# An mLSTM kernel takes its first log rows by products in place of row transfers, and its later logs behind the second unit

## What is computed

```
for t in range(S):
    m_new = maximum(f[t] + m, i[t])
    f_stab, i_stab = exp(f[t] + m - m_new), exp(i[t] - m_new)
    m = m_new
    C = f_stab * C + i_stab * outer(v[t], k[t])
    n = f_stab * n + i_stab * k[t]
    y[t] = sigmoid(o[t]) * (C @ q[t]) / max(|n @ q[t]|, 1)
x = y as (1536, 320)
x = sum over 4 experts e of p[:, e] * (relu(x @ w1[e]) @ w2[e])     # F = 1024
out = ((x @ w_a) * (x @ w_b)) @ w_out                              # 1536 wide
```

## Time and profile before

| what | before |
|---|---|
| median of three runs | 607.03 us (605.69 to 608.39) |
| profiled execution, its own time | 606.54 us |
| its span in the profile | 604.5 us |
| TensorE busy (matmuls) | 597.0 us, 99% of the span |
| VectorE busy | 360.0 us, 60% |
| ScalarE busy | 293.7 us, 49% |
| GpSimd busy | 179.2 us, 30% |
| traffic | 38.38 MB, mean 63 GB/s |

### The profile page before, as it was taken

How to read it: one execution, slowest core, us unless ns; L and a number is a source line. 1 busy time by engine, 2 the same in 40 slices (tenths; PEclk the granted TensorE clock), 3 DMA queues, 4 the chain that set the end, 5 groups by cost and what they waited for, 6 DMA issues and landing times.

```text
span 604.5 us, 10937 instructions
## 1 busy us (share of the span) xinstructions
PE 597.0 (99%) x3991; PEld 581.0 (96%) x3991; DVE 360.0 (60%) x705; ACT 293.7 (49%) x622; POOL 179.2 (30%) x246
## 2 busy tenths in 40 slices
PE   7999999999999999999999999999999999999997
PEld 6888899999999999999999999999999999999997
DVE  7877984454474443644544635389796665666555
ACT  5888745424443344433344434656744543444332
POOL 3466430014340134200425101515035521553000
PEclk9999999999999999999999999999999999999999
DMA  4675541003311011410032100212102310120011
GB/s 128 200 227 183 166 127 51 11 1 69 97 40 62 1 47 23 137 40 23 0 71 87 57 12 1 47 25 87 57 12 47 108 58 12 42 51 1 1 67 65
DMA packets 21028, 38.38 MB, mean 63 GB/s; under 512 B 3520, under 2 KB 11280, under 8 KB 20976
## 3 DMA queue, kind: packets, MB, share of 16 engines
q1 hardware_dynamic: 19040, 35.02, 20.0%
q10 hardware_dynamic: 1936, 2.67, 1.3%
HBM read 26.42 MB, written 1.97 MB: 47 GB/s over the span
## 4 chain that ended last, share of the span: by engine, by line
PE 94%; DVE 4%; issue 1%; DMA 1%; ACT 0%; DVEq 0%
PE PS L1697 38%; PE PS L1616 12%; PE PS L1619 12%; PE PS L1617 12%; PE PS L1618 12%; PE PS L1559 3%; PE PS L1528 1%; PE PS L1516 1%; PE PS L1476 1%; PE PS L1502 1%; PE PS L1478 1%; PE PS L1542 1%; DMA dec_r<-llo 1%; DVE pt L1067 0%; DVE acc L1274 0%
## 5 line engine op out<-in xcount | busy, mean ns | idle before, releaser
L1697 PE MATMUL PS<-w2h,hh 128*128 128x320 f32 x528 | 164.9, 312 | 0.0
L1697 PE MATMUL PS<-w2l,hh 128*128 128x320 f32 x528 | 163.4, 310 | 0.0
L1697 PE MATMUL PS<-w2h,hl 128*128 128x320 f32 x528 | 163.2, 309 | 0.0
L1616 PE MATMUL PS<-xop,wop 128*128 128x384 f32 x400 | 138.5, 346 | 0.0
L1619 PE MATMUL PS<-xop,wop 96*128 96x384 f32 x400 | 135.0, 337 | 0.0
L1617 PE MATMUL PS<-xop,wop 128*128 128x384 f32 x400 | 134.8, 337 | 0.0
L1618 PE MATMUL PS<-xop,wop 128*128 128x384 f32 x400 | 134.6, 337 | 0.0
L734 ACT ACTIVATE hh<-c_s 128x384 fp32r<-128x384 f32 x120 | 62.8, 524 | 100.1 <-DVE c_s L1247 27.9
L1697 PEld LDWEIGHTS PS<-w2h,hh 128*128 128x128 f32 x528 | 99.5, 189 | 0.3 <-DVE hl L1224 0.2
L1697 PEld LDWEIGHTS PS<-w2l,hh 128*128 128x128 f32 x528 | 99.7, 189 | 0.0
L1697 PEld LDWEIGHTS PS<-w2h,hl 128*128 128x128 f32 x528 | 99.4, 188 | 0.0
(11 more groups left out here) (146 smaller groups left out, 803.5 us busy)
## 6 DMA issues: line engine op xcount, KB each, us to landing
s<-in_wt SPq DMA_DIRECT2D x24, 256.0 KB, 3.1
kvo<-in_tok SPq DMA_DIRECT2D x12, 480.0 KB, 4.2
wop<-t1h SPq DMA_DIRECT2D x48, 112.0 KB, 2.2
qk<-in_qk_t SPq DMA_DIRECT2D x24, 160.0 KB
s<-in_w SPq DMA_DIRECT2D x12, 320.0 KB, 2.9
wop<-t1l SPq DMA_DIRECT2D x24, 112.0 KB, 2.2
s<-in_w_out SPq DMA_DIRECT2D x12, 160.0 KB, 2.2
out_y<-acc SPq DMA_DIRECT2D x12, 160.0 KB, 1.9
```

The costliest lines, as they stand in the source:

```text
L1616: nc.tensor.matmul(to, ws[0], xs[0], start=opens, stop=False, skip_group_check=True)
L1697: got = nc.tensor.matmul(bank, left, (w2l if part == 1 else w2h)[p][:, f, :], start=opens and part == 0, stop=closes and part == 2)
```

## The change

Chunk 0's logs are computed first, on 128 columns, and then chunk 1's (`early_logs`). Units 0 and 1 get their row terms without transfers: `log_weights` adds, for each of the 8 heads of such a unit, one product of the head's selecting columns (`dec_r`, 64 partitions) with `lrow`, a tile whose partitions 0 to 15 hold the high and 32 to 47 the low rows. The four transfers of first rows go, and load_rows(2) waits for chunk 1's rows alone. The scan for the rest of the maxima moves behind weigh(0); rest_logs and rest_ends move behind take_num(0) and add_update(0) in unit 1, and normalise(0) behind weigh(2). The halves of m_r move: on SyncE behind load_rows(3), on ScalarE behind weights(1). On TensorE log_weights(0) comes ahead of products(0), log_weights(2) behind update(0), and turning the rest of the logs behind from_state(2); of 17 products of ones 10 stay. On GpSimd the step matrices of chunks 2 to 5 are made after chunk 1's rows, the mask before. load_kvo(1) comes right behind load_qk(1).

```diff
@@ -96,8 +96,9 @@
         li0 = sb("li0", [BH, EARLY], F32, inner)
-        lhi0 = sb("lhi0", [BH, EARLY], F32R, inner)
-        llo0 = sb("llo0", [BH, EARLY], F32R, inner)
+        lf0 = sb("lf0", [BH, P], F32, inner)
+        lrow = sb("lrow", [64, EARLY], F32R, inner)
+        lhi0, llo0 = lrow[0:BH, :], lrow[32:32 + BH, :]
         gate_r = sb("gate_r", [REST, 2, P], F32, inner)
@@ -121,7 +122,6 @@
         inter_s = [sb(f"inter_s{b}", [P, H, D1], F32, inner) for b in range(B)]
-        lf0 = wgt[B - 1][1][0:BH, 0:2, :].rearrange("r c t -> r (c t)")
         num = [sb(f"num{b}", [P, H, D1], F32, inner) for b in range(B)]
@@ -339,7 +339,7 @@
                 c, b = u // B, u % B
-                sp.wait_ge(rows_ready, 1 if c == 1 else 2)
+                sp.wait_ge(rows_ready, 2 if c == 1 else 3)
                 sp.wait_ge(dec_done, 2 * (u - B) + 2)
@@ -348,15 +348,9 @@
-            def load_first_high_row(b):
-
-                sp.wait_ge(rows_ready, 1)
-                sp.wait_ge(picked, 3 * b + 3)
-                sp.dma_start(f32(dec_r[b][64:65, :, :]), f32(lhi0[b * H:(b + 1) * H, 0:P])).then_inc(rows_in[b], 16)
-
             def load_dec_l(c):
-                sp.wait_ge(pool_const, 6)
+                sp.wait_ge(pool_const, 11)
                 sp.wait_ge(dec_l_ready, 1)
@@ -399,21 +393,19 @@
-            sp.dma_start(gate[:, :, 0:EARLY], gates[:, :, 0:EARLY]).then_inc(gates_in, 16)
-            sp.dma_start(gate[:, :, EARLY:S], gates[:, :, EARLY:S]).then_inc(rest_in, 16)
+            sp.dma_start(gate[:, :, 0:P], gates[:, :, 0:P]).then_inc(gates_in, 16)
+            sp.dma_start(gate[:, :, P:S], gates[:, :, P:S]).then_inc(rest_in, 16)
             sp.wait_ge(qk_zero, 1)
...
             load_qk(1)
-            load_first_high_row(0)
-            load_first_high_row(1)
-            sp.wait_ge(m_ready, 1)
-            sp.dma_start(m_r[:, 1, :], m[:, P + 1:S + 1]).then_inc(m_in, 16)
             load_kvo(1)
...
             load_rows(3)
+            sp.wait_ge(m_ready, 1)
+            sp.dma_start(m_r[:, 1, :], m[:, P + 1:S + 1]).then_inc(m_in, 16)
             load_qk(2)
@@ -456,12 +448,17 @@
             nc.gpsimd.memset(ones[:, :], 1.0).then_inc(pool_const, 1)
-            nc.gpsimd.memset(f32(dec_l[:, :, :]), 1.0).then_inc(pool_const, 1)
-            pool.wait_ge(pool_const, 5)
-
-            nc.gpsimd.affine_select(out=dec_l[:, :, :], in_=dec_l[:, :, :], compare_op=ALU.is_ge, fill=0.0, base=PICKED - 1,
-                                    pattern=[[0, NC], [1, P]], channel_multiplier=-1).then_inc(pool_const, 1)
-            pool.wait_ge(rows_ready, 1)
+            nc.gpsimd.memset(f32(lrow[:, :]), 0.0).then_inc(pool_const, 1)
+
+            def steps(cs):
+
+                nc.gpsimd.memset(f32(dec_l[:, cs, :]), 1.0).then_inc(pool_const, 1)
+                pool.wait_ge(pool_const, 6 if cs.start == 0 else 10)
+
+                nc.gpsimd.affine_select(out=dec_l[:, cs, :], in_=dec_l[:, cs, :], compare_op=ALU.is_ge, fill=0.0, base=PICKED - 1,
+                                        pattern=[[0, cs.stop - cs.start], [1, P]], channel_multiplier=-1).then_inc(pool_const, 1)
+
+            steps(slice(0, 2))
             nc.gpsimd.memset(mask[:, :, :], 0.0).then_inc(mask_ready, 1)
@@ -470,6 +467,9 @@
                 nc.gpsimd.memset(vx[b][:, :, D:D1], 1.0).then_inc(pool_const, 1)
+            pool.wait_ge(rows_ready, 2)
+            steps(slice(2, NC))
+            for b in range(B):
                 nc.gpsimd.memset(state[b][:, :, :, :], 0.0).then_inc(pool_const, 1)
@@ -656,12 +656,6 @@
-            def load_first_low_row(b):
-
-                act.wait_ge(rows_ready, 1)
-                act.wait_ge(picked, 3 * b + 3)
-                nc.scalar.dma_start(f32(dec_r[b][65:66, :, :]), f32(llo0[b * H:(b + 1) * H, 0:P])).then_inc(rows_in[b], 16)
-
             def take_v(u):
@@ -779,22 +773,20 @@
                 pick_heads(b)
-            for b in range(B):
-                load_first_low_row(b)
-            act.wait_ge(m_ready, 1)
-            nc.scalar.dma_start(m_r[:, 0, :], m[:, P:S]).then_inc(m_in, 16)
             weights(0)
...
             weights(1)
+            act.wait_ge(m_ready, 1)
+            nc.scalar.dma_start(m_r[:, 0, :], m[:, P:S]).then_inc(m_in, 16)
             gates_of(0)
...
                     weights(u + 1)
-                if u == 1:
+                if u == 2:
                     act.wait_ge(ex_turned, 2)
@@ -1082,7 +1074,7 @@
                 else:
-                    dve.wait_ge(pool_const, 10)
+                    dve.wait_ge(pool_const, 13)
                 for j in range(2):
@@ -1149,23 +1141,30 @@
-            def first_logs():
-                dve.wait_ge(dve_const, 1)
-                dve.wait_ge(pool_const, 4)
-                dve.wait_ge(gates_in, 16)
-                nc.vector.tensor_tensor_scan(m[:, 1:EARLY + 1], gate[:, 1, 0:EARLY], gate[:, 0, 0:EARLY], m[:, 0:1], ALU.add, ALU.max).then_inc(logs0, 1)
-                dve.wait_ge(logs0, 1)
-                n = logs_of(gate[:, 0, 0:EARLY], gate[:, 1, 0:EARLY], m[:, 0:EARLY], m[:, 1:EARLY + 1], lf0, lsum0[:, :], li0[:, :], lhi0[:, :],
-                            llo0[:, :], logs0, 1, True)
-                dve.wait_ge(pool_const, 6)
-                first_two = li0[:, :].rearrange("r (c t) -> r c t", c=2)
-                nc.vector.tensor_copy(dec_l[0:BH, 0:2, :], first_two).then_inc(logs0, 1)
+            def early_logs(c, n):
+
+                cols, ends = slice(c * P, (c + 1) * P), slice(c * P + 1, (c + 1) * P + 1)
+                if c == 0:
+                    dve.wait_ge(dve_const, 1)
+                    dve.wait_ge(pool_const, 5)
+                    dve.wait_ge(gates_in, 16)
+                else:
+                    dve.wait_ge(rest_in, 16)
+                nc.vector.tensor_tensor_scan(m[:, ends], gate[:, 1, cols], gate[:, 0, cols], m[:, c * P:c * P + 1], ALU.add, ALU.max).then_inc(logs0, 1)
                 dve.wait_ge(logs0, n + 1)
-                nc.vector.tensor_tensor(dec_l[32:32 + BH, 0:2, :], first_two, f32(dec_l[0:BH, 0:2, :]), ALU.subtract).then_inc(dec_l0_ready, 1)
+                n = logs_of(gate[:, 0, cols], gate[:, 1, cols], m[:, cols], m[:, ends], lf0[:, :], lsum0[:, cols], li0[:, cols], lhi0[:, cols],
+                            llo0[:, cols], logs0, n + 1, c == 0)
+                dve.wait_ge(pool_const, 7)
+                nc.vector.tensor_copy(dec_l[0:BH, c, :], li0[:, cols]).then_inc(logs0, 1)
+                dve.wait_ge(logs0, n + 1)
+                nc.vector.tensor_tensor(dec_l[32:32 + BH, c, :], li0[:, cols], f32(dec_l[0:BH, c, :]), ALU.subtract).then_inc(dec_l0_ready, 1)
+                return n + 1
+
+            def first_ends():
                 dve.wait_ge(dec_l0_ready, 1)
-
                 nc.vector.tensor_scalar(li0[:, 0:P], li0[:, 0:P], lsum0[:, P - 1:P], None, ALU.add).then_inc(ex_logs, 1)
-                dve.wait_ge(rest_in, 16)
+
+            def rest_maxima():
                 nc.vector.tensor_tensor_scan(m[:, EARLY + 1:S + 1], gate[:, 1, EARLY:S], gate[:, 0, EARLY:S], m[:, EARLY:EARLY + 1], ALU.add, ALU.max).then_inc(m_ready, 1)
@@ -1194,12 +1193,15 @@
-            first_logs()
+            logged = early_logs(0, 0)
+            first_ends()
+            early_logs(1, logged)
             for u in range(NU):
...
                 if u == 0:
-                    rest_logs()
-                    rest_ends()
+                    rest_maxima()
+                if u == B:
+                    normalise(0)
                 if u >= B:
@@ -1208,7 +1210,11 @@
                         x_low(0, u - 7)
-                    normalise(u - 1)
+                    if u == 1:
+                        rest_logs()
+                        rest_ends()
+                    else:
+                        normalise(u - 1)
                 if u == NU - 1:
@@ -1489,17 +1495,22 @@
                     pe.wait_ge(picked, 3 * b + 3)
-                    pe.wait_ge(pool_const, 6)
+                    pe.wait_ge(pool_const, 7)
+                    pe.wait_ge(rows_ready, 1)
+                else:
+                    pe.wait_ge(rows_in[b], 32 * c)
                 if c < 2:
-                    pe.wait_ge(dec_l0_ready, 1)
+                    pe.wait_ge(dec_l0_ready, c + 1)
                 else:
                     pe.wait_ge(dec_l_in[c], 32)
-                pe.wait_ge(rows_in[b], 32 * (c + 1))
                 pe.wait_ge(mask_ready, 3)
...
                     nc.tensor.matmul(PS[:, DEC + q, :], dec_l[:, c, :], dec_r[b][:, q:H:2, :], start=True, stop=False, skip_group_check=True)
+                    for p in range(NP if c == 0 else 0):
+                        nc.tensor.matmul(PS[:, DEC + q, p * P:(p + 1) * P], dec_r[b][0:64, 2 * p + q, :], lrow[:, 0:P], start=False, stop=False,
+                                         skip_group_check=True)
                 for q in range(2):
@@ -1534,7 +1545,7 @@
                 pe.wait_ge(vx_ready, u + 1)
-                pe.wait_ge(pool_const, 10)
```

(14 more changed lines are left out.)

## The result

The changed kernel took 621.71 us (median of six runs, 611.07 to 633.22) against 606.9 for the kernel before (six runs, 605.69 to 608.39). The ratio, which leaves out the runs above 1.5% over the fastest, is 1.0135 with a 95% interval of 1.0069 to 1.0202. The forecast was 608.3 us in a range of 605.0 to 610.8 and "no measurable change": wrong. The six times themselves are part of the result: 611.07, 615.01, 619.58, 623.83, 628.53, 633.22. The six runs of the kernel before have nothing like this spread.

A forecast was written before the change was run, and what follows sets the result against it. TensorE, busy for 99% of the span, was taken to bound the kernel; the start's gain was outweighed by products(3) coming 1.5 us late: 608.0 against the profiled run, 608.5 against the median, forecast 608.3 us, range 605.0 to 610.8.

The forecast's parts named there:

- Start: TensorE, unit 0: first limit ready at 6.45 us, log_weights(0) starts at 6.5 us, not 10.91.
- The added products: log_weights(0) and log_weights(1): 8 more products each at 0.11 us, making the part 1.8 us at high clock.
- What it uncovers: TensorE ahead of unit 3: log_weights(3) waits for unit 2's exponentials; a gain of 1.1 us is left of 4.4.
- The logs of the rest: VectorE: rest_logs starts at 16.2 us, not 13.69; dec_l_ready comes at 19.25, not 16.85, 2.4 us later.
- SyncE's queue: Behind dec_l_ready: 3.36 us of issue to load_qk(3) at 22.65, then 3.8 us; products(3) 1.5 us later.
- The mark: Start of products(3) on TensorE in unit 3: 26.45 us in place of 24.98, 1.5 us later.
- Afterwards TensorE's own work rules.: TensorE behind products(3): later loads add nothing more to the 1.5 us already lost.
- a rival with the clock in it: Clock low from 8.1 us to the end of log_weights(1): 2.5 us on top of +1.5, 610.8 us; chance 0.15.
- The dummy products: Units 0 and 1: seven products of ones gone, named only as a ground for the clock staying low.
- The port: VectorE's first logs: GpSimd's select and cast stop them for 0.9 us in all, 609.2 us; chance 0.1.
- The range: Whole kernel: 605.0 us, the gain's bottom, to 610.8 us, the clock's rival and run scatter.
- the first rival: SyncE does not bind, TensorE's own order decides: −1.1 us, 605.7 us, or −2.3 with cheaper added products; chance 0.25.

The follow-up runs named there:

- the two traces above: Changed kernel with 6 ones ahead of log_weights(4) and 7 ahead of products(3): 609.56 to 622.80 us; with the 6 alone: 609.60 to 621.43 us.
- the run with 622.80 us above: Profiled run of the changed kernel with 6 products of ones ahead of log_weights(4) and 7 ahead of products(3); its four runs: 609.56, 620.89, 622.74, 622.80 us.
- another kernel: Changed kernel with 13 products of ones at the start in place of 10, both waits of unit 3 left: 614.55 to 625.24 us in six runs.
- a third kernel: Changed kernel with only SyncE's order changed, load_kvo(2) and load_qk(3) ahead of load_dec_l(2): 608.03 us median of ten, ratio 1.0032.
- the last kernel: Changed kernel with rest logs early, SyncE's loads reordered, 13 ones at the start, and log_weights(2) ahead of outputs(0): 607.73 us against the kernel before, ratio 1.0035.

## Why the prediction was wrong, step by step

- **Start.** First log product at 7.04 for 6.5: VectorE's first logs ended at 6.77 for 6.45 (two of its operations were longer beside GpSimd's mask, the sums of 0.46 and 0.36 us that take 0.28 and 0.27 for chunk 1), and 0.27 us lie between. Right in kind.
- **The added products.** 0.147 us each for 0.11; they lie between the bounds of 0.068 and 0.213. With 8 to a unit that is 0.3 us a unit, and the wide product of each half took 0.43 from start to start in place of 0.34: 0.5 us a unit in all. In unit 0 that was hidden by luck. The forecast had the first 1.6 us at low clock, 0.8 us of loss, but in the profiled run the products were at full clock from the first on, so log_weights(0) took 2.33 us for 2.55. log_weights(1) had no such help: 2.36 us for 1.8. It ended at 12.98 for 12.1, outputs(0) at 15.98 for 15.0.
- **What it uncovers.** The wait for unit 2's exponentials came as said: 0.67 us at 18.06, for 0.45 expected at 16.8.
- **The logs of the rest.** `dec_l_ready` at 20.21 for 19.25, against 16.85 before. rest_logs took 2.96 us (3.05 expected) and started at 17.25 for 16.2, right behind add_update(0) (16.54 to 17.22), which waited for update(0): the 1 us by which the units were later. m_r was late as well, but did not bind in this run. The scan of the maxima took 1.70 us beside GpSimd in place of 1.27 (timeline of VectorE, below) and ended at 13.82 for 12.8; SyncE issued its half of m_r at 14.49, behind load_rows(3), and it landed 2.3 us after, at about 16.8.
- **SyncE's queue.** 3.38 us from `load_dec_l(2)` to `load_qk(3)` (20.28 to 23.66) for 3.36; products(3) 4.28 after that for 3.8. The mark came at 27.94 for 26.45, 3.0 us late in place of 1.5. Of the missing 1.5 us, 1.0 was `dec_l_ready` and 0.5 the transfer. The mechanism, its place and its order were right; the size was half.
- **"Afterwards TensorE's own work rules."** This is the step that failed. It carried the shift at full clock to the end, and I had priced the waits of unit 3 as waits only. They cost 3 us as waits and 6 us as the clock: two waits of 1.4 and 1.7 us within 4 us of each other, and then 12.7 us or more at half speed. I had a rival with the clock in it, but only from 8.1 us to the end of log_weights(1), priced at 2.5 us. The runs with a low start are low until 38.7 and 39.7 us in the two traces above, and 12 us slower. That the changed kernel itself had such starts is not in its own trace, which is of a run with a high start; it follows from the experiments and from its run of 619.58 us, whose clock reads 1.00 like that of the run with 622.80 us above. The rows before showed the low spacing at the beginning, so the level itself was in sight; what no row showed was how long it can last.
- **The dummy products.** I counted those taken out as nothing but a condition of that rival. Three of them, put back at the start, take away the 12 us that three runs of four had where unit 3 is filled.
- **The port.** Its rival gave 0.9 us for the first logs; 0.3 came there and 0.4 in the later scan, which did not bind. The Trainium skill (SBUF — State Buffer, SBUF: two separate sides) names the pair of engines and the condition, and the scan of 1.70 us, which starts beside the second of two GpSimd products (11.34 to 12.79), agrees.
- **The range.** Its lower end, 605.0, does not hold the first rival's own price of 2.3 us, which makes 604.5. Nothing hung on it.

```profile
3.57 0.46 DVE L1120 TENSOR_TENSOR lf<-gate,m 16x128 f32<-16x128 f32 x1
...
12.12 1.70 DVE L1168 TENSOR_TENSOR_SCAN m<-gate,m 16x512 f32<-16x512 f32 x1
...
17.25 0.48 DVE L1120 TENSOR_TENSOR lf_r<-gate_r,m_r 80x128 f32<-80x128 f32 x1
```

The Trainium skill (TensorE: Matmul & The Clock Gate, What's actually happening) has the lower level as the default and activity as what lifts it. The runs here agree with that much: in the kernel with 13 ones and both waits filled the work from unit 0 on is at full clock, with no wait over 0.67 us. They disagree with reading it as "busy is enough": in the stretch from 28.00 to 40.70 above TensorE is busy for 12.70 of 12.70 us at 0.50.

## What to carry to other kernels

Ahead of TensorE's steady work, price a new wait twice: as the wait, and as the clock that it may cost behind it. In the traces here the clock stayed low for 7 to 31 us, although TensorE was busy. Before taking out products that nothing uses, look at what they stand between, and judge such a change by the spread of its runs and not by one profile. A step moved later on one engine is paid where its results go through a queue: here the 2.4 us that I had counted became 3.4, with five issues and 3.4 us of SyncE between them and the transfer that was waited for.

## What the runs showed of the hardware

- Waits of 1.42 and 1.66 us, and in another kernel of 1.16 and 1.42 us, about 1 us apart, were followed by a granted clock of 0.50 in the profiled runs. By the mean clocks (0.972 to 0.989) it fell in all six runs of the second. Waits of 0.94 and 1.25 us did the same in a third kernel, and a wait of 1.07 us by itself in a fourth. With 6 ones in place of the first wait and 0.88 us left of the other, no run of five shows it. Ones in place of the second wait alone were not tried.
- Once low, the clock stayed there for 13.7 us in the profiled run of the changed kernel and for 30.7 us in that of the one with ones ahead of log_weights(4), although TensorE was busy all along but for 0.56 us in the second, with products of 41 to 512 columns. The shortest such stretch was 6.8 us, in the last kernel.
- Runs of one kernel on one chip differ by 12 us for the same code: 609.60 and 621.40 us, with 10 ones at the start and the first wait of unit 3 filled.
- A product of 64 rows and 128 columns on float32r operands with its own load costs 0.147 us; the score passes of the same size, which take turns between two halves of the rows, cost 0.068.
